# Last segment's second products with the gates as weights, the result by tokens in four shared banks

## What is computed

```python
x = attn_out.reshape(B * S, D)                 # 8192 tokens x 192
h = x @ w_in;  g = np.maximum(0.01 * h, h);  x = g @ w_out
h = x @ w_in2; r = np.maximum(h, 0.0); g = r * r; out = g @ w_out2
```

## Time and profile before

| | us |
|---|---|
| median of 3 runs | 1121.15 (1121.07 to 1121.29) |
| profiled execution, first to last instruction (span) | 1119.2 |
| TensorE matmul busy | 1114.3 (9906 matmuls) |
| TensorE weight load busy | 1080.9 |
| VectorE busy | 874.6 |
| ScalarE busy | 654.9 |

### The profile page before, as it was taken

One profiled execution on the slowest core, in us unless ns is written; L12 is line 12 of the kernel. 1 busy time (PEld: TensorE's weight loads), 2 busy tenths in 40 slices (PEclk: granted clock), 3 DMA queues, 4 the chain that ended last, 5 costly groups with the idle time before them and its releaser, 6 DMA issues.

```text
span 1119.2 us, 22845 instructions
## 1 busy us (share of the span) xinstructions
PE 1114.3 (100%) x9906; PEld 1080.9 (97%) x9906; DVE 874.6 (78%) x1053; ACT 654.9 (59%) x785; POOL 8.5 (1%) x15
## 2 busy tenths in 40 slices
PE   9999999999999999999999999999999999999998
PEld 8999999999999999999999999999999999999998
DVE  8998886978769787786977869878697786975575
ACT  6666656565565565646656565564656656566564
POOL 2000000000000000000000000000000000000000
PEclk9999999999999999999999999999999999999999
DMA  5311010200102001020010200102001010000001
GB/s 167 115 43 55 14 56 2 54 17 15 55 1 58 11 16 55 3 58 9 15 55 6 58 8 16 55 8 58 5 15 54 11 55 5 16 15 15 2 1 29
DMA packets 81203, 36.54 MB, mean 33 GB/s; under 512 B 58452, under 2 KB 78674, under 8 KB 81104
## 3 DMA queue, kind: packets, MB, share of 16 engines
q1 hardware_dynamic: 81104, 35.10, 11.9%
HBM read 23.25 MB, written 6.29 MB: 26 GB/s over the span
## 4 chain that ended last, share of the span: by engine, by line
PE 99%; DVE 0%; DMA 0%; ACT 0%; issue 0%; ACTq 0%; DVEq 0%
PE h_pair L1149 46%; PE y_main_psum L1195 31%; PE y_rest_psum L1199 21%; PE h_pair L1158 0%; PE h_pair L1094 0%; DMA tap_logits<-in_weight_gen_dram 0%; PE y_main_psum L1094 0%; DVE tap_product L730 0%; PE y_rest_psum L1223 0%; PE h_pair L1244 0%; DVE x_windows L965 0%; ACT x_windows L595 0%; DVE tap_sum L710 0%; DVE h_pair L716 0%; DVE tap_shifted L704 0%
## 5 line engine op out<-in xcount | busy, mean ns | idle before, releaser
L1149 PE MATMUL h_pair<-x_parts,w_in_parts 64*128 64x512 f32 x4590 | 563.5, 386 | 0.0
L1149 PEld LDWEIGHTS h_pair<-x_parts,w_in_parts 64*128 64x128 f32 x4590 | 505.6, 184 | 14.7 <-DVE w_in_parts L682 0.2
L1195 PE MATMUL y_main_psum<-g_hi,w_out_parts 64*128 64x512 f32 x2040 | 431.1, 386 | 0.0
L919 DVE TENSOR_TENSOR g_lo<-g,g_hi 128x1024 fp32r<-128x1024 f32 x255 | 311.1, 1220 | 122.6 <-ACT g_hi L581 96.0
L569 ACT ACTIVATE g_hi<-h_pair 128x1024 fp32r<-128x1024 f32 x125 | 128.5, 1028 | 193.4 <-PE h_pair L1149 193.3
L581 ACT ACTIVATE g_hi<-g 128x1024 fp32r<-128x1024 f32 x127 | 134.7, 1061 | 170.5 <-DVE g L910 170.5
L1195 PEld LDWEIGHTS y_main_psum<-g_hi,w_out_parts 64*128 64x128 f32 x2040 | 224.9, 184 | 6.5 <-issue 0.2
L1199 PE MATMUL y_rest_psum<-g_lo,w_out_parts 64*128 64x512 f32 x1020 | 215.5, 386 | 0.0
L1199 PE MATMUL y_rest_psum<-g_hi,w_out_parts 64*128 64x512 f32 x1020 | 215.5, 386 | 0.0
L1195 PE MATMUL y_main_psum<-g_lo,w_out_parts 64*128 64x512 f32 x1020 | 215.5, 386 | 0.0
L910 DVE SCALAR_TENSOR_TENSOR g<-h_pair,u 128x1024 f32<-128x1024 f32 x127 | 155.2, 1222 | 37.9 <-ACT u L575 36.1
(11 more groups left out here) (123 smaller groups left out, 429.8 us busy)
## 6 DMA issues: line engine op xcount, KB each, us to landing
x_windows<-in_x_dram SPq DMA_DIRECT2D x12, 960.0 KB
out_dram<-raw_w_in SPq DMA_DIRECT2D x360, 16.0 KB, 1.5
raw_w_in<-tap_product SPq DMA_DIRECT2D x336, 16.0 KB, 1.8
raw_w_out<-in_moe_w_out_dram SPq DMA_DIRECT2D x16, 192.0 KB, 3.9
tap_logits<-in_weight_gen_dram SPq DMA_DIRECT2D x16, 112.0 KB, 2.9
raw_w_in<-in_moe_w_in_dram SPq DMA_DIRECT2D x8, 192.0 KB, 3.6
raw_w_in<-in_moe_w_in_dram SPq DMA_DIRECT2D x8, 128.0 KB, 3.2
x_windows<-in_x_dram SPq DMA_DIRECT2D x2, 384.0 KB, 4.4
```

The source lines that it names most:

```text
L919: dve.tensor_tensor(GL[n % 4][:, :, :], gate[n % 2][:, :, :], GH[n % 4][:, :, :].bitcast(fp32), ALU.subtract).then_inc(glo_ready, 1)
L1149: last = pe.matmul(h[:, i, :], w[r, slot, a, c], v[r, slot, b, :], start=first, stop=end)
L1195: return pe.matmul(ym[rows][:, :], w[r, c], g[r, i, :], start=start, stop=stop)
```

## The change

Only the downs of segment 31 and what follows them are changed.

`down_by_tokens` takes the gates as the stationary operand, 128 tokens at a time, and streams the weights. A visit v (0 to 31, four for each step) is one of the four blocks of 128 tokens for each half. It has, for each of the 2 blocks of inner numbers and for each half, one matmul of `GH` by 384 columns (high and low weights together) and one of `GL` by 192 columns (high weights). That is 4 pairs a visit, 16 pairs a step.

The result lies by tokens. Each of the four banks (the same four as before, now one tensor `y_banks`) takes one block of 128 tokens: columns 0 to 191 the sum with the high weights, 192 to 383 the sum with the low ones. Both halves add into the same bank, but in different visits: in visit v the lower half works on bank `BANK_ORDER[v % 4]` and the upper on `BANK_ORDER[(v + 2) % 4]`. So a half comes to a bank two visits after the other, and from v = 2 on its first matmul of a visit waits until the other half has finished visit v - 2. Each half signals at its last matmul of each visit.

At the end nothing is folded between banks or transposed. For each pair of banks, ScalarE copies the low columns (2 x 192) to SBUF, and VectorE adds them to the high columns in two operations (2 x 128 and 2 x 64 columns), out of PSUM and into `y_tok`. Banks 0 and 1 are complete after visit 30, banks 2 and 3 after visit 31. SyncE's queue issues two stores of 96 KB for each pair, so four, with 768 bytes for each token.

The downs of the last step wait for all its gates at once, where before the first of its two blocks was waited for alone. The waits for `stored` (that `y_tok`'s memory is free) move to VectorE's first addition.

```diff
@@ PE
+            def down_by_tokens(s, j):
+                n = s * PR + j
+                left = (lower_left, upper_left)
+                pe.wait_ge(glo_ready, n + 1 if j < PR - 1 else n + 2)
+                if j == 0:
+                    pe.wait_ge(y_free, s)
+                for v in range(4 * j, 4 * (j + 1)):
+                    for i in range(2):
+                        for g, width in ((GH[n % 4], 2 * D), (GL[n % 4], D)):
+                            for half, r in enumerate(ROWS):
+                                q = BANK_ORDER[(v + 2 * half) % 4]
+                                if v > 1 and i == 0 and width > D:
+                                    pe.wait_ge(left[1 - half], v - 1)
+                                done = pe.matmul(y_banks[:, q, 0:width], g[r, i, q * P:(q + 1) * P], WO[1][r, j + i * PR, 0:width],
+                                                 start=v < 2 and i == 0 and width > D, stop=v >= VISITS - 2 and i == 1 and width == D)
+                                if i == 1 and width == D:
+                                    done.then_inc(left[half], 1)
...
+                        elif s == SEGS - 1:
+                            down_by_tokens(s, j)
...
-            down(SEGS - 1, PR - 2)
-            last_down()
-            last_turn()
+            for j in range(PR - 2, PR):
+                down_by_tokens(SEGS - 1, j)
@@ ACT
             def last_out():
+                for pair in range(2):
+                    act.wait_ge(lower_left, finished(pair))
+                    act.wait_ge(upper_left, finished(pair))
+                    act.activation(last_low(pair), y_banks[:, 2 * pair:2 * pair + 2, D:2 * D], ACT.Copy).then_inc(last_low_parts, 1)
@@ DVE
             def last_fold():
+                for pair in range(2):
+                    if pair == 0:
+                        dve.wait_ge(stored, BLOCKED * (NCH - 1))
+                    dve.wait_ge(last_low_parts, pair + 1)
+                    rows = y_tok[:, 2 * pair:2 * pair + 2, :]
+                    dve.tensor_tensor(rows[:, :, 0:P], y_banks[:, 2 * pair:2 * pair + 2, 0:P], last_low(pair)[:, :, D - P:D], ALU.add)
+                    dve.tensor_tensor(rows[:, :, P:D], y_banks[:, 2 * pair:2 * pair + 2, P:D], last_low(pair)[:, :, 0:D - P], ALU.add
+                                      ).then_inc(last_summed, 1)
@@ SP
             def store_last(c):
-                sync.wait_ge(last_out_act, 2)
-                sync.wait_ge(last_out_dve, 2)
-                sync.dma_start(out_rows[:, place(c) * (TPC * D):(place(c) + 1) * (TPC * D)],
-                               y_tok[:, :, :].rearrange("p t d -> p (t d)")).then_inc(stored, 16)
+                first = place(c) * TPC * D
+                for pair in range(2):
+                    sync.wait_ge(last_summed, pair + 1)
+                    for q in range(2 * pair, 2 * pair + 2):
+                        sync.dma_start(bass.AP(out.tensor, first + q * BL * TPP * D, [[D, TPC], [TPP * D, BL], [1, D]]),
+                                       y_tok[:, q, :]).then_inc(stored, 16)
```

More of the change, by code:

```diff
@@ L104, in conv_two_ffn_kernel @@
                 made.append(key)
-    PAIR[("last turn",)] = len(made) % 2
-    made.append(("last turn",))
     TURNS = [m for m in made if m[0] != "up"]
@@ L225, in conv_two_ffn_kernel @@
         first_tap_w = hb[1][:, 1, 0:TH * K].rearrange("p (a k) -> p a k", k=K)
-        y_main_pair = pb("y_main_psum", [P, 2, NC])
-        ym = [y_main_pair[:, i, :] for i in range(2)]
-        yr = [pb(f"y_rest_psum{i}", [P, NC]) for i in range(2)]
+        y_banks = pb("y_psum", [P, 4, NC])
+        y_main_pair = y_banks[:, 0:2, :]
+        ym = [y_banks[:, i, :] for i in range(2)]
+        yr = [y_banks[:, 2 + i, :] for i in range(2)]
         first_loaded = [sem("chunk0_last_tokens_loaded"), sem("chunk1_tokens_loaded")]
@@ L277, in conv_two_ffn_kernel, with finished, last_low @@
         y_turned = sem("y_blocks_transposed")
-        last_main_turned = sem("last_y_main_transposed")
         turned_taken = sem("transposed_pair_taken")
[L281 to L300, removed]
+        lower_left = sem("lower_rows_left_bank")
+        upper_left = sem("upper_rows_left_bank")
+        last_low_parts = sem("last_low_parts_copied")
+        last_summed = sem("last_rows_summed")
+        VISITS = 4 * PR
+        BANK_ORDER = (0, 2, 1, 3)
+        def finished(pair):
+            return VISITS - 1 + pair
+        def last_low(pair):
+            return folds[:, pair * 2 * D:(pair + 1) * 2 * D].rearrange("p (q d) -> p q d", q=2)
         block = ctx.enter_context(nc.Block())
@@ L440, in _ @@
                     store_last(c)
-            sync.wait_ge(stored, BLOCKED * (NCH - 1) + 16)
+            sync.wait_ge(stored, BLOCKED * (NCH - 1) + 64)
         @block.gpsimd
@@ L1212, in down @@
                 last.then_inc(down_done, 1)
[L1214 to L1246, removed]
-                for half in range(2):
-                    pe.wait_ge(last_low_copied, half + 1)
-                    pe.wait_ge(last_up_copied, half + 1)
-                    for t in range(half * TPC // 2, (half + 1) * TPC // 2):
-                        for part in (fold_main, y_main):
-                            for i, r in enumerate(ROWS):
-                                last = pe.matmul(last_turned[half][i][:, t % 2 * HP:(t % 2 + 1) * HP], part[r, t * P:(t + 1) * P],
-                                                 ident[r, :], is_transpose=True, start=t % 2 == 0 and part is fold_main,
-                                                 stop=t % 2 == 1 and part is y_main)
-                    last.then_inc(last_main_turned, 1)
```

13 lines of the change are left out of this document (removed).

## The result

The changed kernel has a median of 1124.32 us (1124.28 to 1125.77, 6 runs), the kernel before 1121.18 us (1121.07 to 1121.29, 6 runs). The ratio is 1.003, with an interval of 1.0019 to 1.0042: slower by 3.1 us. The profiled execution took 1124.31 us with a span of 1122.5, against 1119.2 before. I had forecast 1120.8 and a range up to 1123.0.

The account below looks back on a forecast made before the run. TensorE's matmul stream plus the tail bounds the kernel: last matmul ends at 1114.71, tail 4.15 us, span 1118.86 against 1119.2, 0.35 us less, so 1120.8 us. The range was 1119.4 to 1123.0.

Parts of the forecast that it names:

- The chain and the downs: Segment 31's downs: TensorE bounds; narrow pair 0.113 us by the next weights' load, wide 0.173; 18.3 us against 18.16 now.
- the rival of columns alone: Segment 31's downs: weight load needs less than a narrow pair, so downs take 17.0 us, time 1119.5; chance 0.12.
- One sign that I had named: Trace of the downs: narrow to wide start 0.11 us, wide to next 0.17; narrow at 0.09 would mean columns alone.
- Signals and waits: Bank hand-over in segment 31: 60 waits, signals from 9 to 64, all costed at nothing.
- the upper bound of 0.04 us a visit: Segment 31's visits: most that waits and signals together cost, 1.3 us in all, time 1122.1; chance 0.12 as rival.
- the cover of one visit: Bank hand-over: visit v - 1 (0.57 us) hides the release, there 0.31 us after the last pair's start; margin 0.26 us.
- ScalarE and VectorE at the end: Tail: copies of 0.49 us, additions of 0.71 us per bank pair, VectorE late, done 1.42 us after the last matmul.
- The issues: Tail, SyncE's queue: four stores at 0.35 to 0.47 us each, last issued 1.95 us after the last matmul's end.
- The landing: Tail: last 96 KB store lands 1.8 us after issue, taken between 1.5 us (16 KB) and 2.3 us (384 KB).
- The rival on the tail: Final stores: pieces of 768 bytes land no sooner than one of 3072, 0.5 us more, 1121.3; no separate chance given.
- The rival of the hand-over: Bank waits: late release lays bare a 0.11 us load at each of 30 visits, 3.4 us, time 1124.2; chance 0.06.

## Why the prediction was wrong

**The chain and the downs: right.** The TensorE bounds the segment, and a wide and a narrow pair cost 0.284 us, where I had 0.286. That the narrow one is not bound by its columns was shown by taking a third of them away for nothing, so the rival of columns alone is out; that it is the load of the next weights, read from one gap in the earlier trace rows, agrees with this but was not tested by itself. One sign that I had named misleads: the wide pair's row starts 0.09 us behind the narrow one's, which I had given as the mark of columns alone, and the next narrow one 0.19 us later, where I had 0.11 and 0.17. It is the loads that stand 0.11 us apart, and then 0.18:

```profile
1088.37 0.21 PEld L1205 LDWEIGHTS y_psum<-w_out_parts,g_hi 64*128 64x128 f32 x2
1088.48 0.21 PEld L1205 LDWEIGHTS y_psum<-w_out_parts,g_lo 64*128 64x128 f32 x2
1088.66 0.21 PEld L1205 LDWEIGHTS y_psum<-w_out_parts,g_hi 64*128 64x128 f32 x2
```

The sum of both pairs, 0.284 and not 0.266 us, is what tells.

**Signals and waits: right at nothing.** The downs came out at 0.10 us more than before, under my 0.15, so the upper bound of 0.04 us a visit does not show. Nor does the price of about 26 ns for each increment that the Trainium skill has ("TensorE: Matmul & The Clock Gate", section The cost: per-tile semaphore tail). The way to the release is nearer 0.22 than 0.31 us, so the margin under the cover of one visit was larger than my 0.26 us.

**ScalarE and VectorE at the end: right**, 1.29 us against 1.42; VectorE was the late one, with its second pair of sums right behind its first.

**The issues: mis-sized.** I took 0.35 to 0.47 us each from stores that had 128 or 32 outermost. Measured were 0.54 to 0.66. The last issue came at about 1117.5, 2.7 us after the last matmul's end, and not 1.95. On 16 engines they were 0.43 again.

**The landing: the step that failed.** I priced it by size, between 1.5 us for 16 KB and 2.3 us for 384 KB, and called a store of 96 KB nearer to the small one. Both of those rows are stores whose outermost dimension is a multiple of 16. The new one's is 4. The profile gives no time to landing for the new stores; with the same 0.4 us before the end of the span, the last one landed at about 1122.1, an estimate of 4.6 us after its issue at 1117.5, where I had 1.8. The span was missed by 3.6 us (1122.5 against 1118.86): 2.8 of them are this landing, 0.75 the issues, 0.1 the downs' end. The runs with 4, 8 and 128 outermost (1124.3, 1122.5, 1120.7 us) show that the outermost dimension makes the difference, by way of the landing (the data moved for 4.7 us at a share of 0.26) and of the issues. In the sum, with the landing and the issues as on 16 engines, the change measures 1120.72, where I had 1120.8: the other terms were sound. A quarter of the 328 GB/s of the kernel's own last store is 82 GB/s, at which 384 KB take 4.8 us; that was the price to put in. My range had 2.3 us as the landing's end, which covered pieces of another size and not another spread. The rival on the tail had the same blind spot.

The Trainium skill has this rule ("DMA: Bandwidth & Descriptors", section Why a DMA increments its semaphore by 16 and not by 1), and I did not weigh it: a copy issued by SyncE's queue goes over the largest number of engines, 16 at most, that divides the slowest dimension of both its access patterns. All four agree: 4 outermost gives a share of 0.26, 8 gives 0.3 to 0.5, 32 and 128 the short landing. By it the landing alone would have been 512 pieces on 4 engines and the forecast slower. The same section says that the issuing sequencer itself writes the increments of the engines that are not used. That would fit an issue that is longer with fewer than 16 engines: it took 0.56 and 0.63 us on 4 and 8 engines and 0.43 on 16, but fewer engines did not mean a longer issue between 4 and 8, and no run here shows the cause.

**The rival of the hand-over** gave 1124.2 by a mechanism that isn't there. Its agreement with the measured 1124.3 is chance: had I stopped at the time, I would have taken it as shown.

## What to carry to other kernels

Price a store by its bytes divided by the DMA engines it is spread over, and read the spread off the outermost dimension of both sides before taking a duration from another store; keep the partition dimension, or a multiple of 16, outermost (32 and 128 are the ones tried here). The size of the pieces counts for less: by the shares above, an estimate, 3072 bytes take one engine 0.12 us as one piece (0.81 x 16 x 1.2 / 128) and 0.15 us as four (4 x 0.26 x 16 x 4.7 / 512). When results are by tokens in place of features, the order of the tokens within a tile becomes the shape of the last store, and here it was cheapest to set that order where engines with slack copy the input. A rival whose time fits is not yet shown: look for its wait in the trace.

## What was not expected of the hardware

- A store of 128 pieces of 768 bytes on 4 DMA engines moved at about 82 GB/s over four stores in a row (up to 96 in a slice), on 16 engines at up to 296 GB/s in a slice; the 384 KB in four stores on 4 engines cost 3.6 us more at the end of the kernel than on 16.
- The issue of such a store held SyncE's queue for 0.56 us (0.54 to 0.66) on 4 engines, 0.63 (0.60 to 0.72) on 8 and 0.43 (0.35 to 0.43) on 16.
- A moving operand read in pieces of 32 columns cost an up of 9 pairs 0.06 us, 3%.
- The TensorE's release of its own wait came 0.22 us after the start of a matmul of 192 columns, in the one hand-over shown.
